# Opening and drain of a fused attention and two-layer MLP kernel: loads on two queues, idle work, and a later split of x

## The reference, cut to what matters

```python
def _attn_ref(q, k, v, tau):              # q, k, v: 4 x 8 x 576 x 64, fp32
    scale = 1.0 / np.sqrt(q.shape[-1])
    scores = scale * np.matmul(q, k.transpose(0, 1, 3, 2))
    thresh = np.max(scores, axis=-1, keepdims=True) - tau
    scores = np.where(scores >= thresh, scores, -1000000000.0)
    scores = scores - np.max(scores, axis=-1, keepdims=True)
    attn = np.exp(scores)
    attn = attn / (np.sum(attn, axis=-1, keepdims=True) + 1e-09)
    return np.matmul(attn, v)
# x = attention output as 2304 x 512
# layer 1: h = x @ w_in (512 x 2048); r = max(h, 0); g = s * r * r + b; x = g @ w_out
# layer 2: h = x @ w_in; g = max(h, 0) + alpha * min(h, 0); out = g @ w_out
```

## Time and profile before

| | |
|---|---|
| Time, median of 3 runs | 1133.92 us (1133.73 to 1134.54) |
| The profiled execution, whole | 1132.36 us |
| Its span, first to last instruction | 1130.3 us |
| TensorE busy | 1097.9 us (97%) |
| VectorE, ScalarE, GpSimd busy | 527.2 (47%), 510.5 (45%), 262.3 us (23%) |
| Identity matrix ready on GpSimd | 1.48 us |
| First matmul of pair 0, first matmul of layer 1 | 4.52 us, 320.33 us |

### The profile page before, as it was taken

How to read it: one execution, slowest core, us unless ns; L and a number is a source line. 1 busy time by engine, 2 the same in 40 slices (tenths; PEclk the granted TensorE clock), 3 DMA queues, 4 the chain that set the end, 5 groups by cost and what they waited for, 6 DMA issues and landing times.

```text
span 1130.3 us, 18957 instructions
## 1 busy us (share of the span) xinstructions
PE 1097.9 (97%) x5785; PEld 889.0 (79%) x5785; DVE 527.2 (47%) x1008; ACT 510.5 (45%) x941; POOL 262.3 (23%) x440
## 2 busy tenths in 40 slices
PE   6899999999889999999999999899999999999998
PEld 5677777777668888888888889788888888888887
DVE  6788888888633332232233236622332332232232
ACT  4677777777654332232232226633333333333343
POOL 2556556565554400000000008700000000000000
PEclk9999999999999999999999999999999999999999
DMA  6665655655111100000000005400000000000010
GB/s 151 164 158 138 151 143 139 152 134 130 51 38 47 47 19 0 0 0 0 0 0 0 0 0 140 121 1 1 29 9 0 0 37 0 0 37 0 0 38 19
DMA packets 86549, 59.21 MB, mean 52 GB/s; under 512 B 49376, under 2 KB 69872, under 8 KB 86512
## 3 DMA queue, kind: packets, MB, share of 16 engines
q1 hardware_dynamic: 86512, 58.76, 20.3%
HBM read 30.94 MB, written 4.72 MB: 32 GB/s over the span
## 4 chain that ended last, share of the span: by engine, by line
PE 90%; SPq 2%; ACT 2%; POOL 2%; issue 1%; DVE 1%; DMA 1%; ACTq 0%; DVEq 0%
PE psum L836 23%; PE psum L837 23%; PE psum L838 23%; PE psum L954 6%; PE psum L923 6%; PE psum L865 3%; PE psum L867 3%; PE psum L949 1%; PE psum L846 1%; SPq L374 1%; POOL wout_lo L485 1%; POOL win_lo L482 1%; ACT pt L580 1%; PE psum L931 1%; PE psum L920 1%
## 5 line engine op out<-in xcount | busy, mean ns | idle before, releaser
L836 PE MATMUL psum<-x_hi,win_hi 128*128 128x512 f32 (+1 forms) x640 | 238.9, 373 | 1.4 <-DVE x_lo L767 1.4
L837 PE MATMUL psum<-x_lo,win_hi 128*128 128x512 f32 (+1 forms) x640 | 238.4, 373 | 0.0
L838 PE MATMUL psum<-x_hi,win_lo 128*128 128x512 f32 (+1 forms) x640 | 238.4, 372 | 0.0
L836 PEld LDWEIGHTS psum<-x_hi,win_hi 128*128 128x128 f32 x640 | 120.5, 188 | 25.2 <-DVE x_lo L767 2.5
L837 PEld LDWEIGHTS psum<-x_lo,win_hi 128*128 128x128 f32 x640 | 120.6, 188 | 22.9
L838 PEld LDWEIGHTS psum<-x_hi,win_lo 128*128 128x128 f32 x640 | 120.3, 188 | 23.2
L785 DVE SCALAR_TENSOR_TENSOR act_r<-act_n,nalpha,act_r 128x512 f32<-128x512 f32 (+1 forms) x80 | 55.9, 698 | 159.3 <-ACT act_r L638 159.2
L717 DVE SCALAR_TENSOR_TENSOR ex<-psum,thr,ex 128x576 f32<-128x576 f32 x144 | 117.2, 814 | 22.3 <-ACT ex L558 20.0
L774 DVE SCALAR_TENSOR_TENSOR act_r<-act_r,s_c 128x512 f32<-128x512 f32 (+1 forms) x80 | 68.6, 858 | 121.8 <-ACT act_r L627 121.8
L505 POOL TENSOR_SCALAR ex<-ex,none_in,rinv 128x576 f32<-128x576 f32 x144 | 118.5, 823 | 20.1 <-DVE rinv L728 13.6
L777 DVE SCALAR_TENSOR_TENSOR g_lo<-act_r,b_c,g_hi 128x512 fp32r<-128x512 f32 (+1 forms) x80 | 60.2, 752 | 134.3 <-ACT g_hi L630 134.3
(11 more groups left out here) (89 smaller groups left out, 1631.8 us busy)
## 6 DMA issues: line engine op xcount, KB each, us to landing
k_twice<-k_hi SPq DMA_DIRECT2D x64, 144.0 KB, 2.5
stage<-in_moe_w_out_dram SPq DMA_DIRECT2D x32, 256.0 KB, 2.6
out_dram<-stage SPq DMA_DIRECT2D x18, 256.0 KB, 2.2
raw_q<-in_q_dram SPq DMA_DIRECT2D x32, 128.0 KB, 2.4
raw_k<-in_k_dram SPq DMA_DIRECT2D x32, 128.0 KB, 2.6
raw_v<-in_v_dram SPq DMA_DIRECT2D x16, 256.0 KB, 2.6
q_both<-q_hi SPq DMA_DIRECT2D x32, 128.0 KB, 2.3
q_both<-q_lo SPq DMA_DIRECT2D x32, 128.0 KB, 2.3
```

Of the source, the lines that this page charges most:

```text
L836: nc.tensor.matmul(dst, lhs[0], rhs[0], start=first, stop=False)
L837: nc.tensor.matmul(dst, lhs[0], rhs[1], start=False, stop=False)
L838: return nc.tensor.matmul(dst, lhs[1], rhs[0], start=False, stop=final)
```

## The change

The six loads of q and k of pair 1 are issued from ScalarE's queue, as ScalarE's first work; after them ScalarE computes one exponential of a 128x1 column of the identity into `one_exp`, which nothing reads. On SyncE's queue q of pair 2 is loaded right after tau, once q of pair 0 is transposed (`filled` at 1); then come stack(0) and stack(1), then v of pair 0, then k of pair 2, then v of pair 1 and the rest as before. TensorE does 14 transposes of the identity into the o bank before its first step, and 5 more in each step below 4 of the first body (nine steps, 45 transposes), after the step's fill. In the drain, the weight splits move from steps 27 and 28 to 24 and 25, on ScalarE and on GpSimd, and ScalarE's split of x from step 29 to 31, behind the copy of o of step 30.

```diff
--- before.py
+++ after.py
@@ -46,7 +46,6 @@
     LAST = S - (QT - 1) * P
     HALF = S // 2
     G0 = 2 * P
-    UNDER_WAY = 3
     WIDE = 3
     FULL = 2 * (QT - 1)
     TPP = FULL + 1
@@ -91,6 +90,7 @@
         b_c = sb("b_c", [P, 1])
         alpha_rows = sb("alpha_rows", [FC, P])
         nalpha = sb("nalpha", [P, FC])
+        one_exp = sb("one_exp", [P, 1])
 
 
         att = attention_memory
@@ -322,7 +322,7 @@
 
         def drain_step(n0, l):
 
-            return l - BODY - UNDER_WAY if static(n0) and n0 == PAIRS - 2 else None
+            return l - BODY if static(n0) and n0 == PAIRS - 2 else None
 
         def steps(eng, emit):
 
@@ -338,27 +338,33 @@
         block = whole.enter_context(nc.Block())
 
 
+        def load(eng, raw, par, pairs, n, order, landed):
+
+            for h in range(2):
+                eng.dma_start(raw[:, par, 0:QT - 1, D * h:D * h + D],
+                             pairs[bass.ds(n, 1), h, 0:S - LAST, :].rearrange(order, p=P)
+                             ).then_inc(landed, DMA)
+
+        def load_tails(eng, raw, par, pairs, n, landed):
+            eng.dma_start(raw[0:LAST, par, QT - 1, :].rearrange("p (h d) -> p h d", h=2),
+                         pairs[bass.ds(n, 1), :, S - LAST:S, :].rearrange("o h p d -> p (o h) d")
+                         ).then_inc(landed, DMA)
+
+        def load_raw_q(eng, n, par):
+            load(eng, raw_q, par, q_pairs, n, "o (t p) d -> p (o t) d", q_in[par])
+            load_tails(eng, raw_q, par, q_pairs, n, q_in[par])
+
+        def load_raw_k(eng, n, par):
+            load(eng, raw_k, par, k_pairs, n, "o (p t) d -> p (o t) d", k_in[par])
+            load_tails(eng, raw_k, par, k_pairs, n, k_in[par])
+
         @block.sync
         def _(sp):
-            def load(raw, par, pairs, n, order, landed):
-
-                for h in range(2):
-                    sp.dma_start(raw[:, par, 0:QT - 1, D * h:D * h + D],
-                                 pairs[bass.ds(n, 1), h, 0:S - LAST, :].rearrange(order, p=P)
-                                 ).then_inc(landed, DMA)
-
-            def load_tails(raw, par, pairs, n, landed):
-                sp.dma_start(raw[0:LAST, par, QT - 1, :].rearrange("p (h d) -> p h d", h=2),
-                             pairs[bass.ds(n, 1), :, S - LAST:S, :].rearrange("o h p d -> p (o h) d")
-                             ).then_inc(landed, DMA)
-
             def load_qk(n, par):
                 if not (static(n) and n < 2):
                     wait_alone(sp, filled, k_filled(n - 2))
-                load(raw_q, par, q_pairs, n, "o (t p) d -> p (o t) d", q_in[par])
-                load_tails(raw_q, par, q_pairs, n, q_in[par])
-                load(raw_k, par, k_pairs, n, "o (p t) d -> p (o t) d", k_in[par])
-                load_tails(raw_k, par, k_pairs, n, k_in[par])
+                load_raw_q(sp, n, par)
+                load_raw_k(sp, n, par)
 
             def q_filled(n):
 
@@ -412,11 +418,13 @@
 
             load_qk(0, 0)
             sp.dma_start(tau_c[:], tau.partition_broadcast(P)).then_inc(tau_in, DMA)
-            load_qk(1, 1)
+            sp.wait_ge(filled, 1)
+            load_raw_q(sp, 2, 0)
+            stack(0, 0)
+            stack(1, 1)
             load_v(0, 0)
-            stack(0, 0)
-            load_qk(2, 0)
-            stack(1, 1)
+            sp.wait_ge(filled, k_filled(0))
+            load_raw_k(sp, 2, 0)
             load_v(1, 1)
             load_qk(3, 1)
             sp.dma_start(s_c[:], s.partition_broadcast(P)).then_inc(const_in, DMA)
@@ -613,9 +621,13 @@
                     if m == 0:
                         act.wait_ge(win_in, DMA * FC)
                     split_hi(m)
-                if m == IN1_AHEAD:
+                if m == FIRST_OUT - POS + 1:
                     split_x(0, 0)
 
+            load_raw_q(act, 1, 1)
+            load_raw_k(act, 1, 1)
+            act.wait_ge(ident_ok, 2)
+            nc.scalar.activation(one_exp[:], ident[:, 0:1], ACT.Exp)
             steps(act, emit)
 
 
@@ -868,7 +880,7 @@
                                               start=False, stop=True)
                 mm.then_inc(filled, 1)
 
-            OPENING = 4
+            OPENING, QUIET = 4, 4
 
             def fill_scores_unstacked(t):
                 lhs = [x[t.part, t.parity, t.q0:t.q0 + P] for x in (q_hi, q_lo)]
@@ -954,11 +966,18 @@
                     nc.tensor.matmul(o_bank[part, o_cols], raw_v[:, par, h, c, :], pt[:, h, c, cols],
                                      start=(c == 0), stop=False)
 
+            def run_idle(turns):
+                for _ in range(turns):
+                    nc.tensor.transpose(o_bank[:, 0:P], ident[:], ident[:])
+
             pe.wait_ge(ident_ok, 2)
+            run_idle(14)
             pe.wait_ge(padded, PADDED)
 
             def emit(n0, l):
                 fill(Use(n0, l + 2), n0, l + 2)
+                if static(n0) and n0 == 0 and l < QUIET:
+                    run_idle(5)
                 for t in turns_at(n0, l):
                     turn(t)
                 for back in (l % POS, l % POS + POS):
```

## The result

| | before | changed |
|---|---|---|
| Median | 1134.08 us (1133.73 to 1134.73, 6 runs) | 1125.03 us (1124.07 to 1125.84, 6 runs) |
| Ratio to before | | 0.9918 (95%: 0.9906 to 0.9931) |
| Span of the profiled execution | 1130.3 us | 1122.3 us |
| First matmul of layer 1 | 320.33 us | 315.34 us |
| From there to the end | 809.97 us | 806.96 us |

The change is faster by 9.05 us; the ratio's interval corresponds to 7.8 to 10.7 us. I forecast 6.6 us from a time before of 1133.92, with a range that ended at 8.9 (1125.0). The median itself, 1125.03, stands at that end; the gain, against 1134.08, lies just past it. The last two lines of the table say where to look: 4.99 us come from opening and drain together, and 3.01 us come after the first matmul of layer 1, where the change edits nothing. The two profiled executions are 8.23 us apart (1132.36 and 1124.13), 0.82 less than the medians.

A forecast was written before the change was run, and what follows sets the result against it. TensorE is nearly always busy, so only its waits and slow clock can be won, in the opening (SyncE's DMA queue) and drain. 3.8 + 2.95 = 6.75 us off gave 1127.2, stated as 1127.3; range 1125.0 to 1130.8.

The forecast's parts named there:

- The table load ahead of time costs nothing: Opening, ScalarE: the early exponential was taken as free, since one_exp has no reader and it ends near 6 us.
- Opening: Start of attention: SyncE's queue 2.4 to 2.8 us ahead, tile 0 of pair 2 3.8 us sooner, bounds 2.6 to 5.2.
- (3): Opening: k_twice of pair 2 comes last, landing at 46.4 to 46.8; tile 0 of pair 2 near 46.7, not 50.54.
- the 2 us below which I had called the prediction wrong: Opening, sign: the prediction is wrong if SyncE's queue is ahead by less than 2 us at stack(2).
- (1): Opening: tile 0 of pair 1 needs tile 7's PSUM, which VectorE must have masked; it starts near 26.6.
- under 0.5 before 9: Opening, sign on TensorE: transposes of four take under 0.5 us before 9 us.
- Idle work: Opening, TensorE's 14 and 45 idle transposes: taken as 0, bounds 0 and a loss of 1.2 us.
- Drain: End of attention: matmuls with v 1.37 us sooner, 1.59 from the clock, sum 2.95; tile 8 1.35 later.
- Rival (a): Drain: the clock falls all the same, so 1.4 us won in place of 2.95; 1128.9 us, chance 0.24.
- (b): Opening: the two queues do not issue side by side; total gain 2.2 to 4.2 us, centre 1130.4, chance 0.14.
- (c): Opening: idle transposes never raise the level and loads are serial; 2.6 to 3.6 us slower, 1137, chance 0.03.
- (d): Opening: nothing moves, as a later pair waits for the same queue; drain alone gives 1131.0, chance 0.07.

The follow-up runs named there:

- shift32: The kernel before plus one unused 128x1 fp32 tile behind nalpha, so every tile behind it lies 32 bytes further; 1131.76 us, ratio 0.9982.
- opening_only: The changed kernel with the drain put back and without the tile one_exp: the opening alone; 1130.94 us, ratio 0.9982 to before.
- pad64_g: The kernel before with 64 unused bytes ahead of g_hi, so only g and act move; 1137.73 us, ratio 1.0042.
- drain_only: The kernel before with the drain's two hunks alone (weight splits at steps 24 and 25, split of x at 31); 1130.23 us, ratio 0.9970.
- after_noshift: The changed kernel without the tile one_exp, its exponential written to a column of pt_tails; 1127.47 us, ratio 0.9940 to before.
- late_loads: The changed kernel, but ScalarE waits until q of pair 0 has landed before issuing pair 1's six loads; 1130.28 us, ratio 0.9971 to before.
- exp_first: The changed kernel with ScalarE's exponential ahead of its six loads; 1124.50 us, ratio 0.9908 to before.
- no_idle: The changed kernel without any idle transposes (neither the 14 nor the 45); 1125.70 us, ratio 0.9917 to before.

## Why the prediction was right and where it was wrong

**The missing term.** "The table load ahead of time costs nothing: one_exp has no reader" is the step that failed: it put at nothing what was worth 2.0 us. I weighed the instruction and not the declaration. The tile moved 27 tiles, and 8 intervals of a full token tile are 0.26 to 0.29 us shorter each: 2.0 us in the intervals, 1.7 to 2.0 in shift32. Without it the code gives 6.0 to 6.8 us, inside the range. "What follows keeps its order and moves as a whole" was true of the order and not of the pace.

**Opening: mechanism right, size too large.** What came last in the changed kernel was (3), k_twice of pair 2. But SyncE's queue was ahead by 1.31 us at stack(2), less than the 2 us below which I had called the prediction wrong. The forecast was 3.8 us; the profiled executions gave 2.07 at that tile and 2.17 at the end of attention, the time of opening_only 2.5. Two terms were off. First, loads beside loads delay q of pair 0 by 1.0 to 1.2 and k by 1.5 to 1.9, where I had 0 to 0.4 and 0 to 0.8; SyncE was let go at 6.93, not 6.2, and was 1.96 us ahead there (8.89). I had written that two queues ask for 1.26 of the DMA engines, and then taken bounds below what that implies. Second, single issues on SyncE's queue take 0.5 to 1.1 us longer now and then: the three of 18.20 take 2.42 instead of 1.88, the two of 36.84 take 1.74 instead of 0.97 (38.50 before). Together these cost 1.31 us. Before 47 us the profiled execution of before happened to have none; of the nine kernels here with the old opening seven have one.

With the old opening, though, such an issue is not what makes tile 0 of pair 2 late. pad64_g has one (1.53 for a raw_k issue against 0.63) and starts the tile at 50.46, without a wait, as before does (50.54). drain_only starts it at 51.53, also without a wait. What differs is the clock behind the wait of 3.51 us: from 35.6 to 37.2 it is granted 1.00 in before and pad64_g and 0.50 in drain_only and shift32. The four transposes of raw_k of pair 2 show it: 0.60 us at 35.66 before, but in drain_only

```profile
35.76 1.06 PE L846 MATMUL psum<-ident,raw_k 128*128 128x128 f32 x4
```

Over nine kernels with the old opening, the third turn in the drain (306.66 before, in the earlier trace rows's stretch) stood at 306.57 to 307.85, mean 307.17; over seven with the new one at 304.22 to 305.63, mean 305.04. That is 2.1 us.

(1) was right in kind, but late: TensorE waits for the mask of tile 7 and starts pair 1 at 29.53, not 26.6. k of pair 0 came late, and its transposes still ran at the low level: 1.09 us for four at 8.10, where I had given under 0.5 before 9 as a sign.

**Idle work.** I took 0 and bounds of 0 and a loss. It is 0 within the intervals, but not by its cover: it delays tile 0 of pair 0 by 1.1 us (12.62 against 11.54), and both this and the clock that it raises are hidden behind SyncE's queue. The number was right by luck.

**Drain: right, near the numbers.** Forecast 1.35 us lost at tile 8 (309.32 is 1.44 behind 310.05 less 2.17), 1.37 won at the matmuls with v (1.25), 1.59 from the clock (1.57), 2.95 in sum (2.82). Rival (a) is a share of the executions and not another outcome of all of them: after_noshift and the changed kernel have the same waits and 3.75 and 2.37 us.

**Rivals.** (b) fell: while both queues issue, two issues take 1.06 and 1.29 us on ScalarE's and 1.53 on SyncE's, not twice 1.0 to 1.3. That two queues save issue time goes with the Trainium skill's "DMA: Bandwidth & Descriptors", section "Issuing engines are not separate DMA queues": issue time is saved and the transfers share the engines. Its other half, that the transfers interleave, is what cost the opening. The Trainium skill's "Perfetto Trace Analysis", which the prediction cites for (b), names VectorE and SyncE as the two sequencers that share the generator, not ScalarE; so it did not speak for (b), and no run here shows the pair that it names. (c), slower, and (d), nothing won in the opening, fell too: the opening alone wins 2.0 to 2.5 us.

**The sum.** In the profiled executions 2.2 + 2.8 of the code are 5.0 of the forecast 6.75, and the place adds 2.0. That the two make 7.0, near 6.75, is luck: an opening taken too large and a place not seen. Another 1.0 of their difference is the short tile. The median gained 9.05, which is 1 to 2 us more than opening_only, drain_only and shift32 give together (2.5 + 3.2 + 1.7 = 7.4); the intervals of these four reach over that. The profiled execution of before was 1.72 us under its median and that of the changed kernel 0.90, so the rows show less than the medians do; where the rest lies stays open.

## What to carry to other kernels

A new tile in the middle of the declarations is a change of every tile behind it: declare it last, or move it in a kernel of its own and time that first. Where a queue's issue time binds, moving loads to a second queue wins their issue time, but what is needed first should not share the DMA engines with what is needed later. A bare wait ahead of the later loads is no cure: late_loads got q back and lost some 6 us; other work of ScalarE stood behind them. An operation brought forward on an engine that waits for another's result pulls a queue with it: check what stands behind the wait, on GpSimd as on ScalarE.

## What the runs showed of the hardware that I had not expected

- The start-to-start time of fp32 matmuls of 512 columns goes by where their tiles lie in the on-chip memory: 0.2310 us at the old place, 0.2303 with 32 bytes, 0.2266 with 64, 0.2300 with 96, 0.2278 with 128 (tile divided by 384), and 0.2333 in layer 2 with only g and act moved. It repeats to about 0.02 us a tile from kernel to kernel with the same places, and was worth 14 us of 1134.
- Two DMA queues issue side by side, and the loads of both then load the engines. The windows of the changed kernel and of before, from 3 to 4 us, with DMA share and GB/s at the end:

```profile
3.00:4.00 1.00, 1.00 (x7) 1.00 (x6) 0.76 (x4) 0.00 (x0) 0.00 (x0) 1.00 1.24 278
```

```profile
3.00:4.00 1.00, 0.00 (x0) 0.00 (x0) 0.76 (x4) 0.00 (x0) 0.00 (x0) 1.00 0.44 98
```

- ScalarE's DMA queue issued during its table load (exp_first: 1.53, within 1.33 to 2.61).
- TensorE's level after waits of 0.91 and 1.75 us with 0.9 us of work between differs from execution to execution: 1.00 granted in the changed kernel, 0.62 on the mean in after_noshift, 0.64 in late_loads. In no_idle the matmuls of the first group with v ran low (0.52 granted) behind waits of no more than 0.77 us (3.63 us for 16 of 256 columns, 1.95 elsewhere).
- When the level comes back differs too. Behind the old opening's long wait at 28 to 32 us, the raw_k transposes of pair 2 near 35.6 took 0.60 us in three of nine kernels, 0.90 to 1.06 in six. The four at 1.06 start tile 0 of pair 2 at 51.17 to 51.53, the three at 0.60 at 50.35 to 50.54.
